# Attention scores by quarters of the array, with keys side by side, logits ahead of the values and weight splits beside other tiles

## The reference

```
batch, n_heads, seq, head_dim = (4, 8, 768, 64);  n_sink, window = (4, 128)
scores = q @ k.T / sqrt(64)
keep   = (key < n_sink) | ((0 <= query - key) & (query - key < window))
a      = softmax(where(keep, scores, -1e9));   attn = a @ v
...
x = attn as 3072 tokens x 512;  logits = x @ w_gate;  e = argmax(logits)
y = gate * (relu(x @ w1[e]) @ w2[e])          (8 experts, 512 -> 1024 -> 512)
h = y @ w_in;  g = h - tanh(h);  out = g @ w_out   (512 -> 2048 -> 512)
```

## Time and profile before

| | us |
|---|---|
| timed runs, median of 3 | 1077.38 (1075.28 to 1077.5) |
| the profiled execution | 1071.83 |
| its span | 1070.1 |
| tiles 2 to 5 | 12.44 to 39.52 |
| tiles 8 to 11 | 52.26 to 79.64 |
| tiles 14 to 17 | 92.02 to 120.16 |
| tiles 20 to 22 | 132.55 to 154.86 |
| attention's last tile (23) starts | 154.86 |
| experts start | 183.93 |

### The profile page before, as it was taken

One profiled execution on the slowest core, in us unless ns is written; L12 is line 12 of the kernel. 1 busy time (PEld: TensorE's weight loads), 2 busy tenths in 40 slices (PEclk: granted clock), 3 DMA queues, 4 the chain that ended last, 5 costly groups with the idle time before them and its releaser, 6 DMA issues.

```text
span 1070.1 us, 17027 instructions
## 1 busy us (share of the span) xinstructions
PE 1058.0 (99%) x5919; PEld 866.1 (81%) x5919; DVE 651.6 (61%) x1393; ACT 474.8 (44%) x1013; POOL 504.2 (47%) x522
## 2 busy tenths in 40 slices
PE   9999999999999999999999999999999999999997
PEld 6777777888888888888888888888888888888885
DVE  7898895343343434443498666766666666676664
ACT  7988885242143333441644333333333333333332
POOL 4575674661070725770654453444335335344532
PEclk9999999999999999999999999999999999999999
DMA  9647634543142516462411110100101011000001
GB/s 309 205 140 249 215 129 144 197 132 125 51 168 90 197 56 213 169 221 64 140 50 60 51 40 0 42 17 23 30 11 40 11 31 40 1 1 21 20 1 40
DMA packets 38491, 100.16 MB, mean 94 GB/s; under 512 B 8464, under 2 KB 9104, under 8 KB 33296
## 3 DMA queue, kind: packets, MB, share of 16 engines
q1 hardware_dynamic: 29680, 52.68, 15.7%
q0 software_dynamic: 8448, 46.27, 12.2%
q10 hardware_dynamic: 288, 0.26, 0.1%
HBM read 76.06 MB, written 23.13 MB: 93 GB/s over the span
## 4 chain that ended last, share of the span: by engine, by line
PE 91%; DVE 5%; issue 2%; DMA 1%; POOL 1%; ACT 0%; POOLq 0%; DVEq 0%
PE bank L875 24%; PE bank L883 24%; PE bank L818 14%; PE bank L804 14%; PE bank L527 3%; PE bank L565 2%; PE bank L810 2%; PE bank L542 2%; DVE prob L1188 2%; PE bank L791 1%; DVE probT L1204 1%; DMA sorted_x<-x_tok,dest 1%; PE bank L859 1%; PE bank L687 1%; PE bank L589 0%
## 5 line engine op out<-in xcount | busy, mean ns | idle before, releaser
L1673 POOL TENSOR_TENSOR weights<-raw,weights 128x1024 fp32r<-128x1024 f32 x70 | 166.6, 2399 | 187.3 <-ACT weights L943 178.0
L883 PE MATMUL bank<-weights,gT_hi 128*128 128x512 f32 x768 | 238.7, 392 | 0.2 <-DVE gT_lo L1539 0.2
L1796 POOL TENSOR_SCALAR ser<-ser 128x512 f32<-128x512 f32 x96 | 61.6, 642 | 281.0 <-DVE ser L1484 280.9
L875 PE MATMUL bank<-mT_hi,weights 128*128 128x512 f32 x768 | 189.8, 389 | 0.7 <-ACT mT_hi L1112 0.7
L875 PEld LDWEIGHTS bank<-mT_hi,weights 128*128 128x128 f32 x768 | 144.1, 188 | 30.8 <-ACT mT_hi L1112 0.9
L883 PEld LDWEIGHTS bank<-weights,gT_hi 128*128 128x128 f32 x768 | 142.6, 188 | 29.4 <-DVE gT_lo L1539 0.7
L883 PE MATMUL bank<-weights,gT_lo 128*128 128x512 f32 x384 | 149.7, 390 | 0.0
L1126 ACT ACTIVATE bank<-bank 128x512 f32<-128x512 f32 x96 | 55.9, 582 | 210.1 <-DVE ser L1515 210.1
L818 PE MATMUL bank<-weights,hT_hi 128*128 128x512 f32 x448 | 143.5, 401 | 0.0
L804 PE MATMUL bank<-weights,mT_hi 128*128 128x512 f32 x448 | 140.8, 395 | 0.0
L1798 POOL TENSOR_SCALAR sq<-sq 128x512 f32<-128x512 f32 x94 | 140.5, 1495 | 0.0
(11 more groups left out here) (188 smaller groups left out, 1581.8 us busy)
## 6 DMA issues: line engine op xcount, KB each, us to landing
raw<-w_all POOLq DMA_DIRECT2D x32, 1024.0 KB, 5.4
raw<-w_all SPq DMA_DIRECT2D x8, 1024.0 KB, 7.2
sorted_y<-ys SPq DMA_DIRECT2D x30, 261.0 KB, 3.1
xs<-sorted_x SPq DMA_DIRECT2D x29, 261.0 KB, 2.8
v_in<-vt SPq DMA_DIRECT2D x24, 256.0 KB, 3.7
kT<-kt SPq DMA_DIRECT2D x23, 264.0 KB, 3.8
qT<-qt SPq DMA_DIRECT2D x23, 256.0 KB, 4.5
raw<-sorted_y SPq DMA_DIRECT2D x20, 261.0 KB, 2.6
```

Of the source, the lines that this page charges most:

```text
L875: done = e.matmul(bank[HB[n % 3]][:, :], wt[:, f // 2, c, cols], x[:, c, :], start=(m == 0), stop=(m == 3 * CH - 1))
L883: done = e.matmul(bank[YB[i]][:, :], x[:, n % 3, rows], wt[:, f, :], start=(f == 0 and m == 0), stop=(f == GCH - 1 and m == 2))
L1673: e.tensor_tensor(lo, src, hi.bitcast(F32), ALU.subtract).then_inc(s_w_lo, 1)
L1796: e.tensor_scalar(row, row, SERIES_2, 1.0, ALU.mult, ALU.add).then_inc(s_ser, 1)
```

## The change

**Scores.** In tiles with t > 1 each head's matmul becomes two, for queries 0 to 63 and 64 to 127, each of 196 columns: the keys that its queries can see. They use the left and the right column half of the array, so that with two heads there are four quarters. Both heads' banks are waited for before the first of the four. The part of the bank that is not written holds old scores; the mask hides them.

**Keys.** `kT` has for each pair the six tiles of a batch side by side (ring of 6, 132 each), so a head's keys before, sinks and own keys are one run of 260 columns. A load writes four pieces a partition. There is one mask for t > 1 and no `own_first`. The first tile uses 128 columns.

**Order.** `logits` stands ahead of `values` on PE. On ACT `sinks_evict` stands behind two exps in place of three, ahead of `part`.

**Tables.** The high splits of the first expert go from tiles 4, 5, 6, 6, 12, 12, 18, 18 to 4, 5, 6, 8, 9, 10, 11, 12; the low splits from 5, 6, 8, 9, 14, 15, 20, 21 to 5, 6, 11, 11, 12, 12, 17, 18; the last raw load from tile 23 to 20; the scatters of the first two batches from 1, 1 and 4 tokens' tiles in three successive tiles to 2, 2 and 2.

```diff
-    RING_Q, RING_K, RING_V, RING_X = 3, 4, 5, 2 * TILES
+    RING_Q, RING_K, RING_V, RING_X = 3, TILES, 5, 2 * TILES
-    HI_IN, LO_IN, RAW_AT = (4, 5, 6, 6, 12, 12, 18, 18), (5, 6, 8, 9, 14, 15, 20, 21), (16, 17, 18, 23)
+    HI_IN, LO_IN, RAW_AT = (4, 5, 6, 8, 9, 10, 11, 12), (5, 6, 11, 11, 12, 12, 17, 18), (16, 17, 18, 20)
...
-        def keys_of(g, h):
...
+        def keys_of(g, h, first, last):
+            at = g % TILES * HALF
+            return kT[D * (h % 2):D * (h % 2) + D, h // 2, at + first:at + last]
...
-                e.dma_start(kT[:, g % RING_K, :, :].rearrange("p a n -> p (a n)"), kt[g, :, :]).then_inc(k_in[g % RING_K], 16)
+                at = g % RING_K * HALF
+                e.dma_start(kT[:, :, at:at + HALF], kt[g, :, :].rearrange("p (a n) -> p a n", a=PAIRS)).then_inc(k_in[g % RING_K], 16)
...
-                cols = HALF if t == 0 else COLS
-                for h in (2 * pair, 2 * pair + 1):
-                    rows = slice(D * (h % 2), D * (h % 2) + D)
+                heads = (2 * pair, 2 * pair + 1)
+                for h in heads:
                     if H * g + h >= 4:
                         e.wait_ge(s_masked, H * g + h - 3)
-                    e.matmul(bank[S_BANK[h % 4]][:, 0:cols].rearrange("p (n c) -> p n c", c=HALF),
-                             qT[rows, g % RING_Q, pair, :], keys_of(g, h), start=True, stop=True).then_inc(s_scores, 1)
...
+                for n in range(2):
+                    for h in heads:
+                        done = e.matmul(bank[S_BANK[h % 4]][n * HP:(n + 1) * HP, n * HP:COLS - HP + n * HP],
+                                        qT[D * (h % 2):D * (h % 2) + D, g % RING_Q, pair, n * HP:(n + 1) * HP],
+                                        keys_of(g - 1, h, n * HP, COLS - HP + n * HP), start=True, stop=True,
+                                        skip_group_check=True)
+                        if n:
+                            done.then_inc(s_scores, 1)
...
+                if 0 <= w:
+                    logits(w)
                 if in_values:
                     for p in range(PAIRS):
                         values(g, p)
-                if 0 <= w:
-                    logits(w)
...
-                for h in range(3):
+                for h in range(2):
                     exp(i, h)
+                if g >= 0 and g % TILES > 1:
+                    sinks_evict(g)
+                exp(i, 2)
                 if g >= 0 and part_on_act(g, 3):
                     part(g, 3)
-                if g >= 0 and g % TILES > 1:
-                    sinks_evict(g)
...
-                        first = (0, 1, 2, 6) if b < 2 else (0, 3, 6, 6)
+                        first = (0, 2, 4, 6) if b < 2 else (0, 3, 6, 6)
```

More of the change, by code:

```diff
@@ L1187, in masked_max @@
                 e.wait_ge(s_scores, H * g + h + 1)
-                e.tensor_tensor_reduce(row, bank[S_BANK[h % 4]][:, 0:cols], hidden, -SC, 3.0e38, ALU.add, ALU.min,
+                e.tensor_tensor_reduce(row, bank[S_BANK[h % 4]][:, cols], hidden[:, :], -SC, 3.0e38, ALU.add, ALU.min,
                                        negmax[:, g % 2, h:h + 1]).then_inc(s_masked, 1)
@@ L1589, in gpsimd @@
         def gpsimd(e):
-            own = {order: mask[:, order, 1 - order, 0:P] for order in range(2)}
-            prev = {order: mask[:, order, order, 0:P] for order in range(2)}
             step = [0]
```

119 lines of the change are left out of this document (57 added, 62 removed).

## The result

The changed kernel took 1078.68 us in the median of 12 runs (1076.04 to 1080.28), the kernel before on the same chip 1075.76 (1074.01 to 1077.5): a ratio of 1.0023, 95% interval 1.0014 to 1.0032, so 2.9 us slower where 5.0 us faster was forecast, and outside the range. The profiled execution of the changed kernel took 1078.74 us (span 1077.0).

A forecast was written before the change was run, and what follows sets the result against it. PE was taken to bound tiles 2 to 5, DVE 14 to 16 and 20 to 22, ACT 13. Gains 1.9, 0.5, 1.0, -1.0 and 2.6 made 5.0 us, off 1077.4: 1072.4 us, range 1067.5 to 1076.5.

The forecast's parts named there:

- The quarters' block: PE's score block of four heads: quarter matmuls overlap and save 0.28 us a block, 0.55 us a tile.
- rival (c): Score blocks: the array's column halves do not overlap, so the kernel is slower, 1089 us; chance 0.06.
- Tiles 2 to 6: Faster scores on PE gain 0.5 us each in tiles 2 to 4 and 0.4 in 5; 1.9 us.
- Rival (b): Tiles 2 to 6, 8 to 11: the ACT, POOL, DVE loop sets 6.8 us; gain about 1.5, 1075.9; chance 0.14.
- Logits in front: On PE, logits ahead of values: the sinks' eviction lands before the last scores are done; 0 us.
- Keys and masks: Key loads in four pieces stay hidden, taken as 0; narrower masks save 0.1 us in three tiles.
- High splits: ACT's splits moved: tile 7 gains 0.5 us, tiles 8 to 11 1.0, tiles 13 and 19 0.35 each.
- The stall: End of tile 13: DVE waits 4.2 us for POOL's v_sink; tiles 12 to 18 give -1.0 us, not +1.9.
- rival (d): A stall of over 6 us, with the clock falling when PE idles over 2.5 us; about 1079; chance 0.08.
- Tiles 19 to 23: Gains in tile 19, in DVE's idle times of 20 to 22, and in tile 23; 2.6 us together.
- The profile as a measure: The 5.0 us gain comes off both the profiled 1071.8 us and the median 1077.4: 1066.8 and 1072.4.
- tiles 12 to 18 without the stall: Gain of 1.9 us: tile 13 0.35, tile 14 0.3 + 0.57, tile 17 0.5, rest narrower masks and earlier merges.

The follow-up runs named there:

- e10: Kernel before with only the keys side by side and the masks' new arrangement, one wait a pair: 1.0004 of the kernel before.
- e7: Kernel before with only quarters and keys side by side, old tables and order, one wait a pair instead of two: 0.9999 of the kernel before.
- e8: Kernel before with both heads' waits ahead of both score matmuls, 94 wait instructions more on PE: 1.0018 of the kernel before.
- e3: Changed kernel with old tables and old logits' order, so quarters and keys side by side, two waits a pair: 1.0000 of the kernel before.
- e1: Changed kernel with the tables of splits, raw loads and scatters as before the change: 1.0006 of the kernel before.
- e2: Changed kernel with logits behind the values and ACT's sinks eviction behind part 3 again: 1.0024 of the kernel before.
- e9: Kernel before, unchanged, run and profiled again: 1.0009 of itself, profiled execution 1074.14 us.
- e11: Changed kernel with the two low splits at the end of tile 12 moved to tiles 14 and 15: 0.9999 of the kernel before.
- e5: Changed kernel with GpSimd's v_sink copy moved to the end of the batch's first tile, ahead of the low splits: 1.0029 of the kernel before.
- e6: Changed kernel with one wait in place of two before a pair's score matmuls: 1.0037 of the kernel before.
- e17: Changed kernel, unaltered, run and profiled again: 1.0029 of the kernel before.
- e4: Changed kernel with full width scores, one matmul a head over 264 columns: 1.0034 of the kernel before.
- e14: Kernel before with DVE's reciprocal moved behind head 3's masked maximum: 0.9976 of the kernel before.

## Why the prediction was wrong, step by step

**The quarters' block, 0.28 us: right.** 1.09 to 0.83, rival (c) is out.

**Tiles 2 to 6, 1.9 us: wrong, and this is the main step that failed.** The forecast took 0.55 us a tile "less what the second block waits for DVE: it takes 1.15 us, not 1.09". The 1.15 was read in tile 17 and used for tiles 2 to 5, where the second block took 1.30 in the same trace. Behind this stood the reading of the earlier trace rows, that PE, busy throughout, bounds these tiles. A matmul that waits counts as busy there. Measured for the quarters (e10 to e7): 0.15 us in tiles 2 and 3, 0.28 in 4 and 5, 0.9 in all of tiles 2 to 6. In the changed kernel it was 0.08 a tile in 2 to 5, and tile 6 lost more than that. Rival (b) was this, at 0.14; that DVE's idle times there all end on PE, its argument against (b), does not speak against a loop, since PE was waiting for DVE at the same time.

**Logits in front, 0: wrong by 0.3 to 0.8 us.** "That lands before PE has done its last scores" holds in most tiles, not in tiles 0 of a batch with a split ahead (0.51 us in tile 6). One exp went from in front of the eviction; the split ahead of the exps was not looked at.

**The waits of a pair: not in the forecast.** They are in the diff, as a loop of its own over the heads. Alone they cost 1.9 us in the kernel before (e8), 0.7 us of profile with quarters (e3 to e7).

**Keys and masks, 0: right within what can be measured** (e10, 1.0004). In the profile tile 7 gets 0.4 us shorter by them (6.91 to 6.53). The key load's landing isn't late where it counts.

**High splits: wrong in the main.** Tile 7 gained 0.3 us (forecast 0.5), but not by the splits: with the old tables it is as short (6.63 us in e1, 6.53 in e10). Tiles 8 to 11 gained 0.6 (forecast 1.0), of which the tables gave 0.3 (e1 to the changed kernel). Tiles 13 and 19 gained nothing where 0.35 was taken for each.

**The stall: right in place and chain, its cost a little short.** POOL's chain took the 14.2 us of the forecast; DVE waited 3.06 us of it in place of 4.2, since tile 12 had become 0.76 us longer, 0.54 of it through the logits' order (e2). Tile 14 then took 9.71 us, 2.9 over e9's and 3.5 over e11's, where 3.1 less what DVE gets back was taken. The forecast gave it 2.9 us (1.9 without, -1.0 with it); the runs give 2.6 us in the ratio. The clock was in rival (d) only, with PE idle for over 2.5 us. It fell after 2.11 us here, and after 1.95 to 2.74 in e2, e5, e6 and e17, but not after 1.82 in e4; each time for 3.41 us, 1.7 us lost. Rival (d)'s time, 1079, is nearly the measured one; its reason, a stall of over 6 us, is not what happened.

**Tiles 19 to 23, 2.6 us: wrong.** 0.9 against e9 up to tile 23, and tile 23 gave 0.8 back. Of the 1.5 us against the shown profile 0.6 was that profile's own slow tiles.

**The profile as a measure: wrong.** "The difference is not in the attention part that I can see, so I take the gain off both": that was not looked for in the tail. From tile 23 to the end the shown profile takes 3.5 us less than e9 (915.2 against 918.8), by the stall and low clock that it didn't have, and its tiles take 1.2 more. The rest of the 5.5 us goes with the median of only three runs: later medians of this kernel were 1074.3 to 1075.8 us on the chips with the stall. That alone would have left the sum of differences as it was; but on a chip with the stall a part of what quarters gain is lost behind tile 23.

In sum, gains in us, the measured ones by the profiles against e9:

| stretch | forecast | measured |
|---|---|---|
| tiles 2 to 6 | 1.9 | -0.3 |
| tile 7 | 0.5 | 0.3 |
| tiles 8 to 11 | 1.0 | 0.6 |
| tiles 12 to 18 without the stall | 1.9 | -0.3 (e11) |
| the stall | -2.9 | -3.2 (e11 to changed) |
| tiles 19 to 22, and from 23 on | 2.6 | 0.9 and -0.8 |
| sum | 5.0 | -2.8 |

Without the stall 7.9 us were forecast, and the profiles give 0.4; e11's ratio, 0.9999, shows none. In it are 1.1 to 1.8 us of quarters, less what the order, the pairs' waits and tile 23 cost. With the stall it is the result.

## What to carry to other kernels

An engine that is busy for all of a stretch may be waiting inside its instructions: compare the same block at every place where it stands (here 1.09 us in the first half of a tile and 1.30 in the second) before taking the engine for the bound, and read the row in the tile that is priced. Before two engines' work is packed closer, look for instructions of DVE with two SBUF inputs next to long ones of GpSimd; moving the data's arrival doesn't help, only moving the work does. A profiled execution that is faster than all timed runs may come from another chip or another kind of execution: profile the kernel before a second time, beside the timed runs.

## What the runs showed of the hardware

- DVE's subtraction of two SBUF tensors took 3.56 us beside GpSimd's two splits and 0.68 alone, and wasn't let in between the two.
- Four matmuls of 64 by 64 on the four quarters of the array start some 7 ns apart, and 196 columns pass in 0.166 us, with weights changed for each.
- In 15 profiles, 14 of them from four chips, PE finished a run of value matmuls in the tail 1.2 to 3.2 us late (2.3 to 2.4 us of idle time behind it); in the four of another chip never. In e9 counts of PE also rise 0.3 to 1 us late around 78 to 90 us, in e14 none does. What makes it is open; 94 instructions more or fewer on PE don't change it (e6, e7, e8).
- PE's clock fell behind PE's idle stretches of 1.95 to 2.74 us (tile 14, for 3.41 us) and of 2.3 to 2.4 us (tail, for 3.41 or 6.83 us), and stayed at 1.00 behind one of 1.82 (e4).
- DVE's reciprocal waited 0.4 to 1.5 us for a scatter to land in two of the four profiles of one chip and in the shown one of before, in none of 15 others.
- 94 wait instructions more on PE cost the kernel before 1.9 us in 24 tiles (e8), 0.1 us a tile; e3 against e7 shows the same 0.1 us a tile with quarters.
